# Turning q ahead of and behind the sums, and loading the values without their zeros, in a linear-attention front of a fused kernel

## The reference

```
q_s, k_s = q * scale, k * scale          # scale = 64 ** -0.25
phi(x)   = exp(x @ omega.T - |x|^2/2 - max(...)) / sqrt(128)
q_p, k_p = phi(q_s), phi(k_s)            # 576 x 128
kv       = k_p.T @ v                     # 128 x 64
z        = sum over the sequence of k_p  # 128
out      = (q_p @ kv) / (q_p @ z + 1e-6)
```

## Time and profile before

| | |
|---|---|
| median of 3 runs | 771.55 us (771.27 to 772.01) |
| profiled execution | 772.19 us, of which 770.3 us are the span from first to last instruction |
| attention: first matmul to the start of `sums` of unit 15 | 1.60 to 130.94 us |
| of it, steps 2 to 13 (six turns of the loop's pair of steps) | 27.53 to 124.07 us |
| granted TensorE clock, mean | 0.997 of full speed |
| TensorE busy, whole span | 98% |

### The profile page before, as it was taken

How to read it: one execution, slowest core, us unless ns; L and a number is a source line. 1 busy time by engine, 2 the same in 40 slices (tenths; PEclk the granted TensorE clock), 3 DMA queues, 4 the chain that set the end, 5 groups by cost and what they waited for, 6 DMA issues and landing times.

```text
span 770.3 us, 15060 instructions
## 1 busy us (share of the span) xinstructions
PE 756.3 (98%) x5326; PEld 675.5 (88%) x5327; DVE 346.0 (45%) x892; ACT 314.3 (41%) x685; POOL 346.2 (45%) x288
## 2 busy tenths in 40 slices
PE   8999999999999999999999999999999999999996
PEld 7888888888888888888888888998999999999996
DVE  6887878211124435243334346783862331332231
ACT  4888888433242223322243222445324325325220
POOL 6898992344223222222232222258727627528421
PEclk9999999999999999999999999999999999999998
DMA  9888871020040000200020000460172613521121
GB/s 339 297 281 278 287 275 56 29 54 28 1 191 28 1 1 1 109 0 0 0 81 29 1 1 0 143 217 29 32 260 88 213 53 117 172 61 31 31 62 33
DMA packets 26602, 75.30 MB, mean 98 GB/s; under 512 B 3248, under 2 KB 4656, under 8 KB 26432
## 3 DMA queue, kind: packets, MB, share of 16 engines
q1 hardware_dynamic: 22864, 64.13, 23.5%
q0 software_dynamic: 3264, 10.03, 4.3%
q10 hardware_dynamic: 432, 0.59, 0.2%
HBM read 61.11 MB, written 13.63 MB: 97 GB/s over the span
## 4 chain that ended last, share of the span: by engine, by line
PE 85%; DVE 5%; POOL 3%; issue 2%; DMA 2%; ACT 1%; POOLq 0%; SPq 0%; DVEq 0%; ACTq 0%
PE pj L823 26%; PE nm L1035 14%; PE pj L1492 8%; PE tr L1035 6%; PE kv L1035 6%; PE kv L1536 6%; PE nm L1536 6%; PE nm L1492 5%; DMA qk<-in_qk_n 2%; PE pj L311 2%; PE kv L327 1%; DVE pj L580 1%; PE pj L1549 1%; PE nm L389 1%; POOL sqt L231 1%
## 5 line engine op out<-in xcount | busy, mean ns | idle before, releaser
L1008 POOL TENSOR_TENSOR gl<-sg,gh 128x512 fp32r<-128x512 f32 (+1 forms) x80 | 94.9, 1186 | 286.7 <-ACT gh L845 286.7
L839 DVE TENSOR_TENSOR sg<-pj,sg 128x512 f32<-128x512 f32 (+1 forms) x80 | 50.9, 637 | 211.5 <-ACT sg L832 211.4
L832 ACT ACTIVATE sg<-pj 128x512 f32<-128x512 f32 (+1 forms) x80 | 44.2, 553 | 140.2 <-PE pj L823 140.0
L823 PE MATMUL pj<-xh,win_h 128*128 128x512 f32 x256 | 100.0, 391 | 0.0
L823 PE MATMUL pj<-xh,win_l 128*128 128x512 f32 x256 | 99.6, 389 | 0.0
L823 PE MATMUL pj<-xl,win_h 128*128 128x512 f32 x256 | 99.6, 389 | 0.0
L845 ACT ACTIVATE gh<-sg 128x512 fp32r<-128x512 f32 (+1 forms) x80 | 47.2, 590 | 100.1 <-PE tr L1035 61.1
L969 DVE SCALAR_TENSOR_TENSOR raw<-pj,xT 128x512 f32<-128x512 f32 x96 | 62.5, 689 | 20.0 <-ACT pj L910 13.2
L1492 PE MATMUL pj<-xTh,W 128*128 128x288 f32 x320 | 71.3, 300 | 0.2 <-DVE xTl L1751 0.2
L1296 POOL TENSOR_TENSOR W<-wraw,W 128x1024 fp32r<-128x1024 f32 x28 | 66.3, 2399 | 8.2 <-ACT W L1292 8.2
L823 PEld LDWEIGHTS pj<-xh,win_l 128*128 128x128 f32 x256 | 48.1, 188 | 10.1
(11 more groups left out here) (303 smaller groups left out, 1788.1 us busy)
## 6 DMA issues: line engine op xcount, KB each, us to landing
wraw<-in_moe_w SPq DMA_DIRECT2D x7, 2048.0 KB, 10.5
ve<-in_v_z SPq DMA_DIRECT2D x16, 585.0 KB, 4.1
qk<-in_qk_n SPq DMA_DIRECT2D x14, 576.0 KB, 5.8
qkT<-in_qk_t SPq DMA_DIRECT2D x14, 576.0 KB, 6.3
y_rows<-ys SPq DMA_DIRECT2D x18, 256.0 KB, 2.4
stage<-in_moe_w_in SPq DMA_DIRECT2D x8, 512.0 KB, 6.9
y_early<-ys SPq DMA_DIRECT2D x16, 256.0 KB, 3.0
stage<-in_moe_w_out SPq DMA_DIRECT2D x4, 512.0 KB, 5.1
```

Of the source, the lines that this page charges most:

```text
L823: mm = eng.matmul(ph[f % 3][:, 0:tiles_of(n) * P], w[f // F1A][:, c, f % F1A, :], x[:, c, :], start=(c == 0 and w is win_h and x is bh), s ...
L832: eng.activation(sg[f % 2][:, at], ph[f % 3][:, at], ACT.Sigmoid, scale=1.702).then_inc(a_sg, 1)
L839: eng.tensor_tensor(sg[f % 2][:, at], ph[f % 3][:, at], sg[f % 2][:, at], ALU.mult).then_inc(v_g, 1)
L1008: eng.tensor_tensor(gl[f % 3][:, at], sg[f % 2][:, at], gh[f % 3][:, at].bitcast(F32), ALU.subtract).then_inc(g_gl, 1)
```

## The change

Three things:

- **Order.** TensorE's steps 1 to 14 become P0, P1, tq0, sums, P2, tq1, tq2, (tx0, tx1, tx2), out0, out1; step 0 becomes P0, sums, P1, tq0, tq1, tq2, P2, out0, out1. ScalarE's order follows: qf0, b0, kv, qf1, qf2, b1, (x0, x1, x2), [a0], b2, the rest (step 0: kv, b0, qf0, qf1, qf2, b1). The last unit keeps its order.
- **Banks.** tq0, tq1, tq2 write tr, nm0, kv (before: tr, nm0, tr); tx0, tx1, tx2 write tr, nm1, kv (before: kv, nm1, kv). tq2 now waits for kv's copy, tx2 for qf2, and tx0 for qf0.
- **Values.** The host gives v with a column of ones and no zeros (128 rows of 9 x 65). Each unit's ve is loaded by two DMAs of 64 partitions each, into the half of ve that belongs to the head; the other halves are set to zero once, by four memsets on VectorE at the start of the program. `sums` reads its 130 columns as two runs of 65.

```diff
-    ve = [at(f"ve{a}", [P, RJ, VW], 53760 + 4704 * a) for a in range(2)]
+    ve = [at(f"ve{a}", [P, 2, RJ, HW], 53760 + 4704 * a) for a in range(2)]
+    qf_banks = (tr, nm[0], kv)
+    x_banks = (tr, nm[1], kv)
...
         def values(i, a):
             need(eng, p_kv, i - 1)
-            eng.dma_start(ve[a][:, :, :].rearrange("p j c -> p (j c)"),
-                          v_z[bass.ds(i, 1), :, :].rearrange("i p r -> (i p) r")).then_inc(ld_v[a], 16)
+            for b in range(2):
+                rows = slice(HD * b, HD * b + HD)
+                eng.dma_start(ve[a][rows, b, :, :].rearrange("p j c -> p (j c)"),
+                              v_1[bass.ds(i, 1), rows, :].rearrange("i p r -> (i p) r")).then_inc(ld_v[a], 16)
...
-            eng.wait_ge(ld_v[a], 16 * (n + 1))
-            need(eng, a_kv, i)
+            eng.wait_ge(ld_v[a], 2 * 16 * (n + 1))
+            if isinstance(i, int) and i < 2:
+                eng.wait_ge(v_ze, 4)
             if a == 1 and not (isinstance(i, int) and i == 1):
                 need(eng, a_xs, 3 * n)
+            else:
+                need(eng, a_qf, 3 * i)
...
             else:
-                eng.wait_ge(a_qf, 3 * i + 1)
-            bank = nm[0] if g == 1 else tr
+                eng.wait_ge(a_kv, i + 1)
+            bank = qf_banks[g]
...
             if g == 0:
                 eng.wait_ge(v_nm, 2 * OG * (n + 1))
-                eng.wait_ge(a_kv, unit + 1)
+                eng.wait_ge(a_qf, 3 * unit + 1)
             elif g == 2:
-                eng.wait_ge(a_xs, 3 * n + 1)
+                eng.wait_ge(a_qf, 3 * unit + 3)
...
             project(*x, 0)
-            if not (isinstance(i, int) and i == 0):
+            if isinstance(i, int) and i == 0:
+                sums(i, n, a)
                 project(*x, 1)
-            sums(i, n, a)
-            if isinstance(i, int) and i == 0:
+                for g in range(3):
+                    turn_qf(i, n, a, g)
+                project(*x, 2)
+            else:
                 project(*x, 1)
-            turn_qf(i, n, a, 0)
-            turn_qf(i, n, a, 1)
-            project(*x, 2)
+                turn_qf(i, n, a, 0)
+                sums(i, n, a)
+                project(*x, 2)
+                turn_qf(i, n, a, 1)
+                turn_qf(i, n, a, 2)
             if before:
-                turn_x(n - 1, 0, i)
-            turn_qf(i, n, a, 2)
-            if before:
-                turn_x(n - 1, 1, i)
-                turn_x(n - 1, 2, i)
+                for g in range(3):
+                    turn_x(n - 1, g, i)
...
                 copy_kv(i, n, a)
                 exps_b(*x, 0)
+                copy_qf(i, n, a, 0)
             else:
+                copy_qf(i, n, a, 0)
                 exps_b(*x, 0)
                 copy_kv(i, n, a)
-            copy_qf(i, n, a, 0)
             copy_qf(i, n, a, 1)
+            copy_qf(i, n, a, 2)
             exps_b(*x, 1)
             if before:
-                copy_x(n - 1, 0)
-            copy_qf(i, n, a, 2)
-            if before:
-                copy_x(n - 1, 1)
-                copy_x(n - 1, 2)
+                for g in range(3):
+                    copy_x(n - 1, g)
             else:
                 exps_a(*x, 0)
...
     def vector(eng):
+        for a in range(2):
+            for b in range(2):
+                eng.memset(ve[a][HD * b:HD * b + HD, 1 - b, :, :], 0.0).then_inc(v_ze, 1)
```

More of the change, by code:

```diff
@@ L68, in half_steps, with attention @@
         body(i, i // 2, i % 2, i == UNITS - 1)
-def attention(nc, ctx, qk_t, qk_n, v_z, om_2, w_in, w_out, xT, win, wout_a, ident, at, banks, dense):
+def attention(nc, ctx, qk_t, qk_n, v_1, om_2, w_in, w_out, xT, win, wout_a, ident, at, banks, dense):
     win_h, win_l = win
@@ L122, in attention @@
     v_om = sem("v_om")
+    v_ze = sem("v_ze")
     t_qf = sem("t_qf")
@@ L320, in sums @@
             eng.wait_ge(a_exa, PG * i + 2)
-            eng.wait_ge(ld_v[a], 16 * (n + 1))
-            need(eng, a_kv, i)
+            eng.wait_ge(ld_v[a], 2 * 16 * (n + 1))
+            if isinstance(i, int) and i < 2:
+                eng.wait_ge(v_ze, 4)
             if a == 1 and not (isinstance(i, int) and i == 1):
                 need(eng, a_xs, 3 * n)
+            else:
+                need(eng, a_qf, 3 * i)
             for j in range(RJ):
-                mm = eng.matmul(kv[:, 0:VW], feat[a][:, j, :], ve[a][:, j, :],
+                mm = eng.matmul(kv[:, 0:VW], feat[a][:, j, :], ve[a][:, :, j, :],
                                 start=(j == 0), stop=(j == RJ - 1))
@@ L354, in turn_x @@
                 eng.wait_ge(v_nm, 2 * OG * (n + 1))
-                eng.wait_ge(a_kv, unit + 1)
+                eng.wait_ge(a_qf, 3 * unit + 1)
             elif g == 2:
-                eng.wait_ge(a_xs, 3 * n + 1)
+                eng.wait_ge(a_qf, 3 * unit + 3)
             for j in range(3):
-                mm = eng.transpose((nm[1] if g == 1 else kv)[:, j * P:(j + 1) * P],
+                mm = eng.transpose(x_banks[g][:, j * P:(j + 1) * P],
                                    xs[:, 3 * g + j, :, :].rearrange("p h d -> p (h d)"), ident[:, :])
@@ L447, in copy_x @@
         def copy_x(n, g, bank=None):
-            bank = bank if bank is not None else nm[1] if g == 1 else kv
+            bank = bank if bank is not None else x_banks[g]
             eng.wait_ge(t_xs, 3 * n + g + 1)
@@ L1969, in experts_part, with build @@
     return {"sync": sync(), "gpsimd": gpsimd(), "tensor": tensor(), "scalar": scalar(), "vector": vector()}
-def build(nc, qk_t, qk_n, v_z, om_2, moe_w_in, moe_w_out, moe2_w_gate, gate_t, moe2_w1, moe2_w2, out):
+def build(nc, qk_t, qk_n, v_1, om_2, moe_w_in, moe_w_out, moe2_w_gate, gate_t, moe2_w1, moe2_w2, out):
     y_rows = nc.dram_tensor("y_rows", (N, D), F32, kind="Internal").ap()
@@ L2003, in build @@
                            at, ((b0, b1, b2), (nm0, nm1, kv, tr), b3), ahead)
-        attn = attention(nc, ctx, qk_t, qk_n, v_z, om_2, moe_w_in, moe_w_out, xT, win, wo, ident,
+        attn = attention(nc, ctx, qk_t, qk_n, v_1, om_2, moe_w_in, moe_w_out, xT, win, wo, ident,
                          at_attention, (pj, tr, kv, nms), dense)
@@ L2044 @@
 WEIGHTS = ["moe_w_in", "moe_w_out", "moe2_w_gate", "moe2_w1", "moe2_w2"]
-INPUTS = ["qk_t", "qk_n", "v_z", "om_2", "moe_w_in", "moe_w_out", "moe2_w_gate", "gate_t", "moe2_w1", "moe2_w2"]
+INPUTS = ["qk_t", "qk_n", "v_1", "om_2", "moe_w_in", "moe_w_out", "moe2_w_gate", "gate_t", "moe2_w1", "moe2_w2"]
 def laid_out(q, k, v, omega):
@@ L2055, in laid_out @@
     qk_t = qk.reshape(UNITS, P, PG, 2, GT, HD).transpose(0, 3, 5, 2, 4, 1)
-    v_z = np.zeros((UNITS, P, RJ, VW), np.float32)
+    v_1 = np.concatenate([units(v), np.ones((UNITS, P, RJ, 1), np.float32)], axis=3)
     om_2 = np.concatenate([omega.T, omega.T])
[L2058 to L2061, removed]
     return {"qk_t": qk_t.reshape(UNITS, P, T2 * P), "qk_n": qk.reshape(UNITS, P, 2 * RJ * HD),
-            "v_z": v_z.reshape(UNITS, P, RJ * VW), "om_2": om_2}
+            "v_1": v_1.reshape(UNITS, P, RJ * HW), "om_2": om_2}
 def kernel(**inputs):
```

## The result

The changed kernel takes 776.81 us (median of 6, 775.14 to 777.08) against 772.0 us for the kernel before in the same series (771.27 to 772.31): a ratio of 1.0062, 95% interval 1.0051 to 1.0073. It is slower by 4.8 us. Its profiled execution spans 775.1 us.

What follows compares the result with a forecast made beforehand. It took the loop as a ring of dependences with little slack, where queue order decides. 0.7 + 3.0 + 1.6 = +5.3 us on 772.19 gave 777.5, less 0.6 for the profiled execution, taken as 777.0; range 772.0 to 780.5.

Steps and rivals of the forecast that it cites:

- late copies on ScalarE: Leading forecast for attention: q copies behind P2 delay ScalarE's later work; 774.5 to 780 us, chance 0.68.
- qf1 at 4.12, b1 at 4.90: ScalarE, us after P1's end: qf1 begins 4.12 behind tq1; b1, queued behind both copies, 4.90 instead of 3.74.
- Odd step 7.85: Loop's odd steps: P1 needs b2, so 7.85 us against 7.65 before, +0.20.
- The loop's gap of 0.37 us: TensorE, odd step, where the loop turns: 0.37 us between out1 and P0, kept as it is.
- Even step 8.74: Loop's even steps: out1 waits for x1, P1 not for b2; 8.74 us against 8.27, +0.47.
- Six turns +3.0: Units 2 to 13: six pairs of 16.59 us, 99.5 against 96.54 measured, +3.0 us.
- Unit 1 +0.7: Unit 1, an odd step without the loop's gap, P1 held by b2: 7.85 against 7.15 us.
- Unit 14 +1.6: Unit 14: sums of unit 15 needs the late a1, 8.5 us after the start against 6.87.
- Memsets 0: Four memsets on DVE at the start, estimated at 2.4 us, hidden while DVE waits for om_r; 0.
- Loads 0 within 0.5: Value loads: an extra SyncE issue of 0.6 us against 13% fewer bytes, about 0.5; net 0.
- D's mechanism: Rival on loads: two halves land late, qk with them, POOL falls behind; +6 us, 780 to 784, chance 0.10.
- Rival B: Attention loop: ScalarE's slack absorbs the order, removed waits and late squares count; -1.8 to -3.1 us, chance 0.14.

Runs made afterwards that it cites:

- e3: Changed kernel with P2 back behind tq1, old banks, and b1 and x0 back ahead of qf2 on ScalarE; 772.17 us, ratio 1.0005.
- e5: Changed kernel with a0 right behind kv in ScalarE's queue, except in step 0; 774.41 us, ratio 1.0036.
- e8: e5 with tx1 turned first, its copy x1 ahead of b2, and copies x0 and x2 behind b2; 772.42 us, ratio 1.0009.
- e12: Changed kernel with b1 moved ahead of qf1 and qf2 in ScalarE's queue, except in step 0; 776.66 us, ratio 1.0062.
- e4: Changed kernel with the turned output in order tx1, tx0, tx2 and copy x1 ahead of b1; 776.71 us, ratio 1.0060.
- e1: Changed kernel with values loaded as before, in one transfer with zeros; order and banks of the change kept; 775.85 us, ratio 1.0052.
- e2: Kernel before, order and banks kept, with values loaded without zeros in two transfers, plus the memsets; 772.38 us, ratio 1.0007.
- e14: Kernel before with each ve loaded with its zeros, but by two transfers of 64 partitions; 782.99 us, ratio 1.0142.
- e11: Kernel before with values in one transfer without zeros and each head's sums as nine matmuls of 64 rows; 835.24 us, ratio 1.0821.

## Why the prediction was right

It forecast 777.0 us by late copies on ScalarE; 776.81 was measured. The mechanism is the one that was forecast. That the number came within 0.2 us is in part luck: the six turns were taken 1.0 us too long, the start and unit 1 0.7 us too short, and the kernel before took 772.0 us beside the change, not the 771.55 that the sum starts from. By its own steps:

- **qf1 at 4.12, b1 at 4.90.** The mechanism held, in the profile (b1 at 4.69 and 4.70 in the steps shown), by e3, which takes the turns back, and by e5 and e8, which leave the turns behind P2 and win 2.1 and 4.1 us by ScalarE's order (e8 with tx1 first). e12 shows that moving b1 alone ahead of the copies doesn't do it. The size was 0.2 too large: P2 follows sums without the 0.09 us I had put between them (80.69 - 78.59 = 2.10), and qf1 begins 0.58 behind the start of tq1 (81.56, 82.14), not 0.65.
- **Odd step 7.85; it was 7.79.** The path held: P1 goes on when b2 ends, at 6.91 (forecast 7.08; b1 itself came 0.2 earlier than forecast), and behind the pause it takes 0.87, not 0.77. The loop's gap of 0.37 us, which I kept, is gone: P0 starts 0.05 behind out1, perhaps because PE had waited for qf1 meanwhile, which no run tests. It was off the path: P1 waits for b2 all the longer, 0.31 us in place of 0.01. e5 shows that this hold is real: with b2 0.2 earlier the step takes 7.57.
- **Even step 8.74; it was 8.64.** out1 waits for x1 as forecast (0.33 us idle). I had P1 free of b2; e4 showed b2 right behind, so that taking x1's wait away gives 0.13 a step; e5 gives nothing there, and e8, which eases both, 0.38.
- **Six turns +3.0; +2.0 measured.** The difference is the 0.17 us a pair of these two steps.
- **Unit 1 +0.7; +1.05.** e1 has 7.79, so about 0.4 belong to the loads: in both VectorE waits there for the squares, but they come 1.13 us behind the end of P1 in the change and 0.72 in e1, and only in the change does P2 then wait. **Unit 14 +1.6; +1.5,** by a1, as worked out; P2 also waited for b0 until 3.2, as forecast.
- **Memsets 0.** VectorE at the start, answering to the earlier trace rows:

```profile
0.99 0.55 DVE L574 MEMSET ve<- 64x585 f32 x1 [0.99 <-PEq L2083]
...
3.17 0.55 DVE L574 MEMSET ve<- 64x585 f32 x1 [0.18 <-issue]
3.75 0.23 DVE L576 TENSOR_SCALAR om<-om_r 128x128 f32<-128x128 f32 x1
```

Four of 0.55 us each, about 0.72 from one to the next, make om2 0.18 us late (3.75 against 3.57), which nothing waits for: the first projection begins at 4.88, where it began at 4.89. The Trainium skill's one cycle per element (VectorE: DVE Perf Modes, "Zero memsets can be issued as uint32 (trn2)") would be an estimate of 0.61 us each; the row has 0.55, a little less, and the row decides.
- **Loads 0 within 0.5; by the profiles of e1 and the change they cost 0.9,** all of it in the start and unit 1, against the rest of the sum, which was too large. The prediction counted bytes, and gave the two transfers a wrong size (585 KB become 292.5 in all, two of 146). It did not look at the start, where the DMA engines are full, and it took 0.6 us for the second issue where the two together take SyncE 1.15 us (e2) and the one took 0.33. Seven kernels with two transfers ended P1 for unit 2 at 20.0 to 22.2 us, mean 21.1; four with one, at 20.2 to 20.4. Against that, the loop of the change and, behind its first pair, of e2 has no late squares; e3 and e8 still have some. In the timed runs this comes to 1.0007 for e2, and to 1.0062 against 1.0052 for the change with and without, both within the intervals. So D's mechanism (the halves late, qk with them, GpSimd behind) is there at the start, and far smaller than its 6 us. The Trainium skill's advice against two transfers to disjoint halves (DMA: Bandwidth & Descriptors, "Rules for kernel authors") holds here, and with rows of 4680 bytes more strongly than serial halves would make it, since e14 loses 11 us at equal bytes. Why a split should cost so much with rows of 4680 bytes and little with 2340 is open.
- **Rival B** (ScalarE has slack enough) fell: ScalarE is busy 78.6 of 98.55 us and still sets the time, because its idle 0.98 us lie ahead of tq1's copy, which blocks the ready b1 and a0 behind it in the queue. Its relief, the late squares, came true in e2, whose last five pairs are 0.85 us shorter in all than those of the kernel before; in the changed order it is worth nothing, since e1, with the old loads, has the same steps.

## What to carry to other kernels

When each engine runs its queue in order, a move on one engine is paid on the one whose queue interleaves with it: write down the times at which each instruction of that queue becomes ready, before and after, and look for the idle time ahead of the first late one. If a wait is taken away and nothing comes of it, look for a second hold of the same size (against the kernel before in each series, the change loses 4.8 us, e4 5.0, e5 2.7 and e8, which eases both holds, 0.7). Count transfers and not bytes alone wherever the DMA engines are already full, and above all at the start.

## What the runs showed of the hardware

- Loading the same 585 KB by two transfers of 64 partitions in place of one of 128 raised the busy share of the DMA engines from 0.79 to 0.92 between 30 and 120 us, at 277 and 272 GB/s, and the time by 11 us.
- A matmul of 64 rows and 65 columns, behind others on the same 64 rows, took 0.12 us (4.33 us for 36, as the profile counts them), as long as one of 128 rows and 130 columns (2.11 us for 18). 18 weight loads of 128 columns took 2.09 us in both.
- In e11, with these matmuls, the granted clock of TensorE, 0.997 on average before, fell to 0.953, in stretches such as 82.58 to 87.56 us (0.86, so partly the 1.2 GHz level); TensorE was busy 99% of the whole span, and from 73.19 to 77.52, ahead of that stretch, 4.27 of 4.33 us at 1.00.
- SyncE took 0.33 us to issue one transfer of 128 partitions for ve, and 1.15 us to issue the two of 64 (e2, at 64.78 us).
